# Attention feeding two mixer layers on one core: the first batch's probabilities are transposed three heads behind their scores, not two, and multiplied by the values five heads behind, not four

## The reference, cut to what matters

```python
def _attn_ref(q, k, v, n_sink, window):          # q, k, v: batch 2, heads 8, seq 768, head_dim 64
    scores = scale * np.matmul(q, k.transpose(0, 1, 3, 2))
    keep = is_sink | in_window                   # 4 sink keys, or within 128 positions back
    scores = np.where(keep, scores, -1e9)
    a = np.exp(scores - np.max(scores, axis=-1, keepdims=True))
    return np.matmul(a / (np.sum(a, axis=-1, keepdims=True) + 1e-09), v)

def _moe_ref(x, U, V, w_ch1, w_ch2):             # x: (2, 768, 512); the second mixer has w_tok1, w_tok2
    h = x.transpose(0, 2, 1) @ U @ V             #   with a relu between for U, V
    u = x + h.transpose(0, 2, 1)
    return u + np.maximum(u @ w_ch1, 0.0) @ w_ch2
```

## Time and profile before

| what | value |
|---|---|
| median of 3 runs | 631.31 us (630.80 to 631.43) |
| the profiled execution | 630.87 us, its span 628.8 us |
| TensorE busy in the span | 614.8 us (98%) |
| VectorE, ScalarE, GpSimd busy | 351.8, 323.9, 402.3 us |
| granted TensorE clock | 1.00 of full speed in all 40 slices |
| batch 0's heads on TensorE | from 9.68 us to 75.11 us of the span |

### The profile page before, as it was taken

One profiled execution on the slowest core, in us unless ns is written; L12 is line 12 of the kernel. 1 busy time (PEld: TensorE's weight loads), 2 busy tenths in 40 slices (PEclk: granted clock), 3 DMA queues, 4 the chain that ended last, 5 costly groups with the idle time before them and its releaser, 6 DMA issues.

```text
span 628.8 us, 10350 instructions
## 1 busy us (share of the span) xinstructions
PE 614.8 (98%) x3462; PEld 555.1 (88%) x3462; DVE 351.8 (56%) x755; ACT 323.9 (52%) x726; POOL 402.3 (64%) x425
## 2 busy tenths in 40 slices
PE   7899999999999999999999999999999999999997
PEld 6788889999999989999999888899998888999986
DVE  6676664554564646776657731495667227665411
ACT  4666666555555556654544444544453447454321
POOL 7676557978979775665665744567566537666352
PEclk9999999999999999999999999999999999999999
DMA  8482333554343525313232332432324332421252
GB/s 173 93 183 52 87 99 103 134 123 115 92 109 98 154 71 154 99 63 118 85 95 91 116 95 85 122 102 68 117 84 118 115 121 84 150 84 35 51 160 73
DMA packets 88467, 65.59 MB, mean 104 GB/s; under 512 B 43040, under 2 KB 72480, under 8 KB 88416
## 3 DMA queue, kind: packets, MB, share of 16 engines
q1 hardware_dynamic: 88416, 64.95, 37.3%
HBM read 61.52 MB, written 3.15 MB: 103 GB/s over the span
## 4 chain that ended last, share of the span: by engine, by line
PE 87%; DVE 4%; issue 3%; ACT 3%; POOL 2%; DMA 1%; DVEq 0%; ACTq 0%; SPq 0%
PE bank L1624 34%; PE bank L1374 23%; PE bank L1589 10%; PE bank L1450 4%; PE bank L1420 3%; PE bank L1553 3%; PE bank L1503 3%; PE bank L1430 2%; PE bank L1529 1%; PE bank L1397 1%; POOL w_lo L882 1%; DVE masked L1145 1%; PE bank L1616 1%; ACT probs L901 1%; PE bank L1484 1%
## 5 line engine op out<-in xcount | busy, mean ns | idle before, releaser
L882 POOL TENSOR_TENSOR w_lo<-w_raw,w_hi 128x512 fp32r<-128x512 f32 (+1 forms) x158 | 210.5, 1339 | 138.1 <-ACT w_hi L915 137.1
L915 ACT ACTIVATE w_hi<-w_raw 128x512 fp32r<-128x512 f32 (+1 forms) x158 | 96.6, 618 | 54.2 <-PE bank L1624 35.9
L1624 PE MATMUL bank<-w_hi,hid_hi 128*128 128x512 f32 x216 | 86.4, 400 | 0.0
L1624 PE MATMUL bank<-w_hi,hid_lo 128*128 128x512 f32 x216 | 85.0, 394 | 0.0
L1624 PE MATMUL bank<-w_lo,hid_hi 128*128 128x512 f32 x216 | 84.8, 392 | 0.0
L901 ACT ACTIVATE probs<-masked,neg_max 128x264 f32<-128x264 f32 x96 | 49.4, 515 | 65.4 <-DVE neg_max L1145 65.0
L1624 PE MATMUL bank<-w_hi,y_hid 128*128 128x512 f32 x216 | 71.1, 394 | 0.2
L1145 DVE CUSTOM_DVE_ANT_0 masked<-bank,masks 128x264 f32<-128x264 f32 x96 | 40.7, 429 | 30.3 <-PE bank L1420 27.0
L1450 PE MATMUL bank<-v_nat,probs_T 128*128 128x64 f32 x352 | 50.7, 263 | 3.6 <-DVE probs_T L1164 2.4
L1450 PEld LDWEIGHTS bank<-v_nat,probs_T 128*128 128x128 f32 x352 | 47.9, 190 | 5.8 <-DVE probs_T L1164 3.6
L1624 PEld LDWEIGHTS bank<-w_hi,y_hid 128*128 128x128 f32 x216 | 40.5, 188 | 9.5 <-POOL w_lo L882 1.5
(11 more groups left out here) (177 smaller groups left out, 1496.0 us busy)
## 6 DMA issues: line engine op xcount, KB each, us to landing
w_raw<-in_moe_w_ch_dram SPq DMA_DIRECT2D x144, 256.0 KB, 2.7
w_raw<-in_moe_w_ch_dram SPq DMA_DIRECT2D x20, 512.0 KB, 3.5
q_nat<-in_q_dram SPq DMA_DIRECT2D x12, 256.0 KB, 3.2
k_nat<-in_k_dram SPq DMA_DIRECT2D x12, 256.0 KB, 4.0
v_nat<-in_v_dram SPq DMA_DIRECT2D x12, 256.0 KB, 3.8
out_dram<-o_stage SPq DMA_DIRECT2D x11, 256.0 KB, 3.3
w_raw<-in_moe_w_tok_dram SPq DMA_DIRECT2D x6, 256.0 KB, 2.7
w_raw<-in_moe_w_tok_dram SPq DMA_DIRECT2D x8, 192.0 KB, 2.3
```

The costliest lines, as they stand in the source:

```text
L882: nc.gpsimd.tensor_tensor(w_lo[:, split % NW, 0:n], w_raw[:, split % NR, 0:n], w_hi[:, split % NW, 0:n].bitcast(f32), ALU.subtract) \
L915: nc.scalar.activation(w_hi[:, split % NW, 0:n], w_raw[:, split % NR, 0:n], ACT.Copy) \
L1624: last = mm(m_tile(use)[:, :], stationary, w[:, slot, :], start=False, stop=(final and n == 2), skip_group_check=True)
```

## The change

The lags of batch 0 become (3, 5). Two steps that were placed by head number move with them: `down` goes from head 6 to head 7 of its tile, and the building of two triangles on GpSimd hangs on `("pv", 7)` where it hung on `("pv", 8)`, which is the same unit, 12. By the same rules `sinksT` falls on head 4 where it fell on head 3, ahead of `ksplit` in that unit's list, and `sinkpv` on head 5. No instruction is added or taken away. Batch 0 has one more unit at its end.

```diff
-    LAGS = {0: (2, 4), 1: (2, 3)}
+    LAGS = {0: (3, 5), 1: (2, 3)}
...
-            if b == 0 and h == 6 and T > 0:
+            if b == 0 and h == 7 and T > 0:
                 now.append(("down", 1, b, T - 1))
...
-                elif s == ("pv", H):
+                elif s == ("pv", H - 1):
                     nc.gpsimd.memset(triangles[:, :, :], 1.0).then_inc(triangles_built, 1)
```

## The result

| kernel | median | executions | ratio to before, 95% interval |
|---|---|---|---|
| before, beside it | 631.04 us | 630.68 to 631.43 (5) | |
| changed | 634.05 us | 633.75 to 636.48 (5) | 1.0054, 1.0043 to 1.0066 |

The change makes the kernel 0.5% slower, 3.0 us, where +0.3 was predicted with a range up to 633.2. Its first profiled execution took 636.48 us (span 634.7) at a mean granted clock of 0.995 and was its longest; a second one, 633.93 us (span 631.9) at 1.000, is what the tiles are read from.

A forecast was written before the change was run, and what follows sets the result against it. TensorE, busy 98%, was taken as the bound, with 8.3 us of first-batch waits on offer; tile terms summed to -0.4 at the low ends and +0.9 at the high, middle +0.3 on 631.31, giving 631.6, range 629.4 to 633.2.

The forecast's parts named there:

- tiles 0 and 1: Up to the first `sinksT`, old waits of 3.3 become 2.3, -1.0; tile 1's second half +0.4.
- tile 4: Old waits 1.8, new 1.3, or 2.1 if GpSimd's second weight part comes between the key casts: -0.5 to +0.3.
- tile 2: New waits 1.0 less old 0.5 (0.31 and a `sinksT`): +0.5.
- tile 3: Old waits 1.1, new 1.0, or 1.6 if head 26's query cast meets GpSimd's splitting of V: 0 to +0.5.
- tile 5 and the end: Tile 5's waits 1.7 less 1.1, +0.6; at batch 0's end two waits for odd copies shrink, -0.4.
- step 1: Tiles 1 to 5: ScalarE's copy of head 1 falls behind head 4's exponential, so its `pv` newly waits 0.9 per tile.
- rival B: Even-copy and `probsT` waits go and head 1's `pv` hardly waits: about -3, 628.3, or 629.8 with half; chance 0.20.
- the sign: Evidence named for the forecast: VectorE idle ahead of line 1168 for 0.4 and more.
- step 2: `kT` and `sinksT`, sharing two banks with odd heads' transposes that ScalarE drains late, wait about 0.1 each.
- step 3: Tile 5: three query casts behind head 38's copy make head 42's `masked` late; `sinksT` waits 0.9, `pv` some 0.7.
- rival C: VectorE casts meet GpSimd splits in tiles 3 and 4, 0.8 each; lines 1103, 1123 near 1.2 repeatedly; 633.2, chance 0.25.
- The product by U: Moving `down` from head 6 to head 7 costs TensorE the same 0.86 in either place.

The follow-up runs named there:

- e6: Changed kernel with first-batch copies swapped (even heads to ScalarE, odd to VectorE) and `sinksT` one unit earlier, on head 3; 629.25 us, 0.9980.
- e1: Changed kernel with only the sinks and sums of a tile one unit earlier, on head 3; 634.24 us, 1.0055.
- e4: Changed kernel with only the first batch's copies swapped: even heads to ScalarE, odd heads to VectorE; 631.25 us, 1.0013.
- e3: Changed kernel with GpSimd's subtraction of tile 6's queries made to wait for all three VectorE casts; 633.06 us, 1.0034.
- e2: Changed kernel with the first two weight chunks back in the units where the kernel before has them; 632.72 us, 1.0028.
- e10: Changed kernel with only the product by U put back in head 6; 633.92 us, 1.0052.
- e5: Kernel before, lags kept at 2 and 4, with only the product by U moved from head 6 to head 7; 631.62 us, 1.0016.
- e9: Changed kernel with copies swapped, sinks on head 3, weight chunks in old units, GpSimd's subtraction behind the casts, product by U in head 6; 630.08 us, 0.9994.
- e11: Changed kernel with copies swapped, sinks on head 3, weight chunks in old units, GpSimd's subtraction behind the casts, run again; 629.46 us, 0.9975.
- e7: Changed kernel with copies swapped, first two weight chunks in old units and GpSimd's subtraction behind the casts; 630.44 us, 1.0000.
- e0: Changed kernel run again without edits, for a second profile; 633.93 us, 1.0057.

## Why the prediction was wrong

Forecast was +0.3, measured +3.0 by medians and +2.3 by traces with like first products. Three terms of the sum failed, and in each the step is named below: in tile 5 the casts were priced as if nothing met them, in tiles 0 and 1 the new waits were taken as 1.0 smaller than the old, and in tile 4 the collision was given only half its weight.

| part | predicted | on the traces |
|---|---|---|
| tiles 0 and 1 | -1.0 + 0.4 = -0.6 | +0.05 |
| tile 2 | +0.5 | +0.6 |
| tile 3 | 0 to +0.5 | 0.0 |
| tile 4 | -0.5 to +0.3 | +0.5 |
| tile 5 and the end | +0.6 - 0.4 = +0.2 | +1.05 |
| sum | +0.3 | +2.3 |

**Right: step 1, the new wait at head 1.** Its nine handovers came within 0.05 us each, tile 2 lost 0.6 where 0.5 was summed, tile 3 came out at its low end, and rival B fell with it. The edit that shows it is e6: with another engine for that copy and `sinksT` in head 3, tile 2 is 0.96 shorter, the whole of the 1.0 summed for its waits. Neither part alone does that (e1 0.04, e4 0.26), so the chain as a whole is shown and no single link. The larger sums that e4 and e6 give back are not this step alone, since both also undo the collision of tile 5. VectorE stood idle ahead of line 1168 for only 0.24 in tile 2, where 0.4 and more was named as the sign; in tile 4 it was 0.62. Of step 2's two bank waits of 0.1, that of `kT` shows as 0.24 in tiles 2 and 3, that of `sinksT` not at all there.

**Wrong: tile 5, step 3.** "`sinksT` waits 0.9 for its bank": 1.87. The step priced three casts at their usual length and did not ask which GpSimd instruction they release. Line 548, whose two parts take 2.81, may start behind the first cast, and the later casts run into it. e3 removes just that: the wait becomes 0.89, and the kernel gets 0.7 back by the traces. With tile 5 and the end 0.85 over the forecast, this is the largest single term, rival C's mechanism at a place that neither C nor the sum had. The Trainium skill, SBUF — State Buffer, section "Who interferes with whom", says that whichever of such a cast and a GpSimd instruction comes first holds the shared port pair for its whole length. The trace agrees: the cast of 1.55 us began 0.01 behind a subtraction of 1.28 and ended 0.28 after it, and the casts take 0.42 once GpSimd is held back.

**Wrong: tile 4.** The collision was foreseen ("if GpSimd's second weight part comes between the two key casts, 2.1") and put at the high end, +0.3. The middle of the range gave it half of that. It happened in both traces. In the second one `sinksT` waits 0.7 and `pv` 1.58, together 2.3, and tile 4 lost 0.5. e2 gives 0.6 back and not more; in its trace the weight split meets the query cast of the same tile (1.31), and `kT` waits 0.67.

**Wrong: tiles 0 and 1.** The waits of before did go, but their place was taken nearly in full: up to head 14's scores the gain is 0.3 (24.52 before, 23.59 in e3, less 0.62) and not 1.0. The +0.4 summed for tile 1's second half came true. `qT` 2 waits 0.85 where 0.5 was summed, scores wait 0.5 for GpSimd's part of the keys, which the sum did not have, and `sinksT` 0 waits 0.6; behind head 14, `pv` of head 1 waits 0.8. The bound was there ("the other end is 0, with every old wait kept under another name") and was not taken into the middle. No experiment took this part by itself, so why these waits are this long stays open. In the quick traces the profile puts the 0.85 of `qT` 2 down to the load of the queries, but it ends 0.37 behind the start of ScalarE's copy in the second trace (17.04, 17.41) and in e3's (16.23, 16.60). That fits a wait for the bank, not for the load.

**The product by U** was put at nothing, and in the changed kernel that is right (e10). It is no property of the step: in e5 moving it took away a cover and cost 0.9, and in e9 it waits 0.54 itself in three tiles when everything else is on time. What the parts are worth depends on each other, so the sum of tiles was only as good as the assumption that each wait stands alone.

**The range** reached to C's 633.2. C's terms (0.8 a meeting, no gain in tiles 0 and 1) made +1.9. The traces account for +2.3, since a meeting lengthens the casts by 1.0 and more; the other 0.7 of the medians' 3.0 is in none of the cases (below). So even C, the nearest case, was too low, and its sign was not met: no more than one cast of lines 1103 and 1123 in a trace lasted 1.2 or more.

## What to carry to other kernels

When a lag in an ordered plan is changed by an odd number, look at which engine serves which parity: the copies that alternate between two engines change their neighbours. Read what such an edit gives back tile by tile: the swap alone gave 1.9, but 1.65 of it in tile 5 and the end, where it undid another collision as well. Here the longer lag beats the kernel before only with the swap and with the sinks' transpose kept in head 3 (0.9980, 0.9971 to 0.9988). And for each cast on VectorE ask which GpSimd instruction it releases, and whether the next cast follows it into that.

## What the runs showed of the hardware

**Long waits of TensorE were followed by a lower clock.** First trace of the changed kernel, stretches of one and two microseconds, columns as in the earlier trace rows, the seventh the granted clock:

```profile
58.00:60.00 2.00, 0.81 (x7) 0.60 (x6) 1.92 (x8) 0.60 (x3) 1.53 (x3) 1.00 0.60 131
60.00:61.00 1.00, 0.67 (x7) 0.67 (x7) 1.00 (x3) 0.78 (x4) 0.59 (x3) 1.00 0.00 0
...
62.00:63.00 1.00, 1.00 (x4) 0.51 (x3) 0.48 (x3) 0.70 (x3) 0.84 (x3) 0.50 0.03 8
```

TensorE had waited 1.74 for tile 4's `pv`; from about 61.9 to 65.1 us it then had 0.50 of full speed, its 1.2 GHz level, and again after tile 5's wait of 1.86 (0.51 in 72 to 74). The second trace, with waits of 1.58 and 1.87, kept 1.00 throughout. The mean clock was 0.997 or less in 5 of 10 executions of the changed kernel, in 2 of 5 of e1 and 3 of 6 of e10, which keep both long waits, in 1 of 5 of e3, and in none of 6 of e2 or of 76 of the kernel before. The two traces of the changed kernel differ by 2.86 at the mixer's first product (87.03 and 84.17), so this is about what the falls cost there. The executions at both of its medians had a clock of 1.000, so the fall is not in the 3.0. Why it comes in one execution and not in another stays open.

**The first products run at one of two paces.** The second trace, from its first scores, and then that of `e3_pool_after_casts`:

```profile
9.52 0.56 PE L1420 MATMUL bank<-k_hi,q_hi 128*128 128x264 f32 x1 [0.28 <-DVE k_lo L563]
9.88 0.42 PE L1420 MATMUL bank<-k_lo,q_hi 128*128 128x264 f32 x1
10.10 0.42 PE L1420 MATMUL bank<-k_hi,q_both 128*128 128x264 f32 x1
```
```profile
9.71 0.36 PE L1422 MATMUL bank<-k_hi,q_hi 128*128 128x264 f32 x1 [0.95 <-DVE k_lo L565]
9.91 0.28 PE L1422 MATMUL bank<-k_lo,q_hi 128*128 128x264 f32 x1
10.03 0.28 PE L1422 MATMUL bank<-k_hi,q_both 128*128 128x264 f32 x1
```

From start to start 0.22 us against 0.12, until about 13.8 us, though the granted clock of that stretch is recorded as 1.00 in both. The Trainium skill, TensorE: Matmul & The Clock Gate, section "Seeing it yourself", warns that the clock's events in traces of trn2 have been seen to be unreliable. These rows agree. From the first scores to head 16's it costs 0.99 (19.01 against 18.02); the slow trace began 0.19 earlier, which leaves the 0.80 above. Executions of most kernels here fall into two groups about 1 us apart (e11: 628.37 to 628.47 and 629.42 to 629.79). The pace goes with the group: e2's trace is slow and of the upper one, and the eight quick traces without a fall of the clock (before, e3 to e7, e9 and e11) are of the lower. So the pace very likely makes the groups.

**The changed kernel's 0.7.** Of 76 executions of the kernel before that ran beside e0 to e11, 55 have spans up to 628.9, the quick group, and 19 have 629.4 to 629.7. The changed kernel's five executions at a clock of 0.999 or more have 631.8 to 632.2, where 628.8 + 2.3 = 631.1 would be expected of a quick one. Group against like group, that is 2.1 to 2.8 about a middle of 2.4, near the +2.3 of the traces. So the medians' 3.0 compares mostly executions with different first products. That the changed kernel has none with quick first products and an undisturbed clock may be the clock's doing: e1's and e10's traces have quick first products and the fall. But the first trace has the fall too and starts at the lower pace (0.22), and e10 has two executions at 1.000 with a span of 631.4. So no link of the two is shown.
